# A decayed-attention stage taken two chunks at a time, followed by a three-pass matmul network

## The chip, the cores and the metric

The kernel runs on one core of a Trainium2 chip. The metric is the time of one execution on the device in microseconds (us): 280.35, the median of 3 runs (280.11 to 280.44). Engines are called as in the profile: PE is the matmul engine, PEld its weight loads, DVE the vector engine, ACT the scalar engine, POOL GpSimd, SP the engine that issues all the transfers here.

## What is computed

Attention over 2 batches, 8 heads, 768 positions and head size 64, without softmax. In the reference a block of 64 positions gives

```
intra = (q @ k.T * Dmask) @ v                  # Dmask[i, j] = lam ** (i - j), lower triangle
inter = (q * lam ** (pos + 1)) @ kv_state
out   = intra + inter
kv_state = lam ** block * kv_state + (k * lam ** (block - 1 - pos)).T @ v
```

and the state of a block goes into the next one. Two dense stages follow on x (1536 x 512). The first shifts by one token: `xk = mu_k*x + (1-mu_k)*x_prev`, `xr` likewise, `k = relu(xk @ w_k)` (512 to 1024), `v = k*k @ w_v`, `x = sigmoid(xr @ w_r) * v`. The second is `(sigmoid(conv5(x)) * (x @ w_val)) @ w_out`. Everything is float32.

## The kernel before

**Attention.** The kernel works in chunks of 128 positions: 6 chunks in each of 2 batches, n = 0 to 11. A chunk has four groups of matmuls on PE: `scores(n)` (S), `update(n)` (U, the product that goes into the state), `inter(n)` (I, query times state) and `attend(n)` (A, weighted scores times v). Chunks 0 and 6 begin a batch and have no I; chunks 5 and 11 end one and have no U. All operands have 64 rows or 64 columns somewhere, so the groups use PE cut into parts: S as 64*128, U and A as 128*64, I as 64*64 (the profile gives this shape in each row). Around them:

- POOL makes `kdec` (keys with decay, `decay_k`, needed by U) and `qd` (queries with decay, `decay_q`, needed by I).
- DVE multiplies the scores with the decay table (`weigh`, pT, two instructions, needed by A) and adds the next state (`new_state`, needed by the next I).
- ACT scales the old state first (`fade`, four instructions, needed by `new_state`) and copies the output of a chunk from PSUM to x (`evacuate_x`, needed before PE writes the same banks again).
- Each engine has one queue, in the order in which the code lists its work. PE's order is S(n+1), U(n), I(n), A(n). In the gaps ACT and DVE already mix the first 512 tokens (`mix_part`, `mix`, `mix_high`, `mix_low`) and split w_k into a high and a low part (`high`, `low`).
- S has two pairs of PSUM banks, U two banks, the output banks 4 and 5 (0 and 1 for the last chunk). kdec, qd, pT and state have two buffers each. Loaded chunks have 6 buffers (`IN_BUFS`), qk and kv of a chunk being one transfer of 512 KB each.

**Dense stages.** Each product is made of three matmuls of 128x512 (`three_pass`: high*high, high*low, low*high). For a block t of 512 tokens `hidden(t, n)` makes 8 groups of 12 matmuls, `receptance(t, m)` 4 groups, `value(t, m)` 4 groups of 24. `hidden(0, 0)` waits for all four pieces of the low part of w_k (`wk_lo` at 4). `receptance` waits for `xr_lo` and the squares that free its banks, `value` for 8 `kk_lo` and 4 `wv_lo`.

Of the kernel before, what the change touches and what calls it, by code (L numbers as in the profile page):

```python
# [29 lines left out]
IN_BUFS = 6  # L30
# [18 lines left out]
def build(nc, prm_in, qk_in, kv_in, w_k, w_v, w_r, w_val, w_out, out):  # L49
    with ExitStack() as ctx:  # L50
# [10 lines left out]
        def place(name, shape, at, dt=F32):  # L61
# [44 lines left out]
        in_at = [kk_at + i * 8 * KB for i in range(4)] + [ring_at, r_at]  # L106
        qk = [place(f"qk_{i}", [P, 2, DM], in_at[i]) for i in range(IN_BUFS)]
        kv = [place(f"kv_{i}", [P, 2, DM], in_at[i] + 4 * KB) for i in range(IN_BUFS)]
        pT = place("pT", [P, 2, 2, DM], xr_at)
        kdec = place("kdec", [P, 2, DM], xr_at + 8 * KB)  # L110
        qd = place("qd", [P, 2, DM], xr_at + 12 * KB)
        dec = place("dec", [P, H, CH], own_at)
        qdec = place("qdec", [P, PAIRS, CH], own_at + 4 * KB)
        state = place("state", [P, 2, PAIRS * D], own_at + 6 * KB)
        faded = place("faded", [P, PAIRS * D], own_at + 8 * KB)
        zeros = place("zeros", [P, CH], own_at + 9 * KB)
        warm = place("warm", [P, P], own_at + 10 * KB)
        spare = place("spare", [P, 1], own_at + 11 * KB)
        ident = place("ident", [P, P], own_at + 12 * KB)
# [5 lines left out]
        ps_s, ps_u = [[ps[:, 2 * i + j, :] for j in range(2)] for i in range(2)], [6, 7]  # L125
# [20 lines left out]
            sem(z) for z in "wk_hi wk_lo wr_hi wr_lo wv_hi wv_lo w2_hi w2_lo".split()]  # L146
        (xk_part, xk_full, xk_hi, xk_lo, xr_part, xr_full, xr_hi, xr_lo) = [
# [23 lines left out]
        def out_banks(n):  # L171

            return (0, 1) if n == NCH - 1 else (4, 5)
# [21 lines left out]
        def _(sp):  # L195
# [22 lines left out]
            load_qk(2)  # L218
            load_kv(1)
            load_qk(3)  # L220
            load_kv(2)
            load_kv(3)
            load_qk(4)
            load_kv(4)
            load_qk(5)
            load_kv(5)
            load_qk(6)
            load_kv(6)
            load_qk(7)
            load_weight(wk_raw, w_k, 0, wk_here)  # L230
            load_kv(7)
            load_qk(8)
            load_kv(8)
            load_weight(wk_raw, w_k, 1, wk_here)
            load_qk(9)
            load_kv(9)
            load_weight(wk_raw, w_k, 2, wk_here)
            load_qk(10)
            load_kv(10)
            load_qk(11)  # L240
            load_weight(wk_raw, w_k, 3, wk_here)
            load_kv(11)
            for i in range(2):
                load_weight(wr_raw, w_r, i, wr_here)
            for i in range(4):
                load_weight(wv_raw, w_v, i, wv_here)
# [19 lines left out]
        def _(pool):  # L266
            def decay_k(n):
                if has_update(n):
                    i = n % IN_BUFS
                    pool.wait_ge(kv_here[i], 16 * (n // IN_BUFS + 1))  # L270
                    if updates(n) > 2:
                        pool.wait_ge(update_done, updates(n) - 2)
                    nc.gpsimd.tensor_tensor(  # L273
                        kdec[:, updates(n) % 2, :].rearrange("p (h d) -> p h d", h=H),
                        kv[i][:, 0, :].rearrange("p (h d) -> p h d", h=H),
                        dec[:, :, CH - 1:CH].to_broadcast([P, H, D]), ALU.mult).then_inc(kdec_ready, 1)

            def decay_q(n):
                b, c = at(n)
                if c > 0:  # L280
                    i = n % IN_BUFS
                    pool.wait_ge(qk_here[i], 16 * (n // IN_BUFS + 1))  # L282
                    if inters(n) > 2:
                        pool.wait_ge(inter_done, inters(n) - 2)
                    nc.gpsimd.tensor_tensor(
                        qd[:, inters(n) % 2, :], qk[i][:, 0, :],
                        qdec[:, :, :].rearrange("p a i -> p (a i)"), ALU.mult).then_inc(qd_ready, 1)
# [11 lines left out]
            decay_k(0)  # L299
            pool.wait_ge(qdec_ok, PAIRS)  # L300
            decay_q(1)
            for n in range(1, NCH):
                decay_k(n)
                if n + 1 < NCH:
                    decay_q(n + 1)
# [4 lines left out]
        def _(act):  # L310
            def evacuate_x(n):
                b, c = at(n)
                cols = slice(b * SEG + HALO + c * CH, b * SEG + HALO + (c + 1) * CH)
                act.wait_ge(att_done, n + 1)
                first = out_banks(n)[0]
                nc.scalar.copy(x[:, :, cols].rearrange("p (g a) i -> p g a i", g=2),
                               ps[:, first:first + 2, 0:2 * CH].rearrange("p g (a i) -> p g a i", a=2)).then_inc(x_ready, 1)

            def fade(n):

                act.wait_ge(state_ready, updates(n - 1))
                for a in range(PAIRS):
                    cols = slice(a * D, (a + 1) * D)
                    nc.scalar.activation(faded[:, cols], state[:, n % 2, cols], ACT.Copy,
# [7 lines left out]
            def mix_part(t, k, which):  # L332

                to, done, free = ((xk_f, xk_part, h_done), (xr_f, xr_part, r_done))[which]
                act.wait_ge(x_ready, min(CT * (t + 1), NCH))
# [69 lines left out]
            evacuate_x(0)  # L405
            act.wait_ge(qdec_ok, PAIRS)
            fade(1)
            evacuate_x(1)
            fade(2)
            evacuate_x(2)  # L410
            fade(3)
            evacuate_x(3)
            fade(4)
            mix_part(0, 0, 0)
            mix_part(0, 1, 0)
            evacuate_x(4)
# [12 lines left out]
            evacuate_x(8)
            fade(9)  # L430
            high(wk, wk_raw, 1, wk_here, wk_hi)
            evacuate_x(9)
            fade(10)
            high(wk, wk_raw, 2, wk_here, wk_hi)
            evacuate_x(10)
            high(wk, wk_raw, 3, wk_here, wk_hi)
            evacuate_x(11)
# [58 lines left out]
        def _(dve):  # L496
            def weigh(n):

                dve.wait_ge(scores_done, n + 1)
                if n >= 2:  # L500
                    dve.wait_ge(att_done, n - 1)
                for row in range(2):
                    nc.vector.tensor_tensor(pT[:, n % 2, row, :], ps_s[n % 2][row],  # L503
# [3 lines left out]
            def new_state(n):  # L507
# [5 lines left out]
                if inters(n - 1) > 0:  # L513
                    dve.wait_ge(inter_done, inters(n - 1))
                to, got = state[:, (n + 1) % 2, :], ps[:, ps_u[updates(n) % 2], 0:PAIRS * D]
# [86 lines left out]
            for n in range(NCH):  # L602
                if n + 1 < NCH:
                    weigh(n + 1)
                new_state(n)
                if n == 4:
                    mix(0, 0, 0)
                    mix(0, 1, 0)
                if n == 5:
                    mix(0, 2, 0)  # L610
                    mix(0, 3, 0)
                if n == 6:
                    mix_low(0, 0, 0)
                if n == 7:
                    mix_low(0, 1, 0)
                    mix_low(0, 2, 0)
                if n == 8:
                    mix_low(0, 3, 0)
                    low(wk, wk_raw, 0, wk_hi, wk_lo)
                if n > 8:  # L620
                    low(wk, wk_raw, n - 8, wk_hi, wk_lo)
            for i in range(2):
                low(wr, wr_raw, i, wr_hi, wr_lo)
# [59 lines left out]
        def _(pe):  # L683
# [23 lines left out]
            def update(n):  # L707
# [7 lines left out]
                if u > 2:  # L715
                    pe.wait_ge(state_ready, u - 2)
                for a in range(PAIRS):
                    for row in range(2):
                        h, at_k = head_of(row, a), (row * PAIRS + a) * D
                        last = nc.tensor.matmul(ps[rows_of(row), ps_u[u % 2], a * D:(a + 1) * D],  # L720
                                                kdec[:, u % 2, at_k:at_k + D], kv[i][:, 1, h * D:(h + 1) * D],
# [3 lines left out]
            def place_of(n, row, a):  # L725
                return ps[rows_of(out_half(row, a)), out_banks(n)[a // 2], a % 2 * P:(a % 2 + 1) * P]

            def inter(n):
# [5 lines left out]
                if n < NCH - 1:  # L734
                    pe.wait_ge(x_ready, n)
                else:
                    pe.wait_ge(p_ready, 2 * n)
                for a in (0, 2, 1, 3):
                    for row in range(2):
                        last = nc.tensor.matmul(place_of(n, row, a), state[rows_of(row), n % 2, a * D:(a + 1) * D],  # L740
                                                qd[rows_of(row), inters(n) % 2, a * P:(a + 1) * P],
                                                start=(a % 2 == 0), stop=False, skip_group_check=True)
                last.then_inc(inter_done, 1)

            def attend(n):
# [4 lines left out]
                if c == 0 and n > 0:  # L750
                    pe.wait_ge(x_ready, n)
                for a in range(PAIRS):
                    for row in range(2):
                        h = head_of(row, a)
                        last = nc.tensor.matmul(place_of(n, row, a), kv[i][:, 1, h * D:(h + 1) * D],  # L755
                                                pT[:, n % 2, row, a * P:(a + 1) * P],
                                                start=(c == 0 and a % 2 == 0), stop=(a % 2 == 1), skip_group_check=True)
                last.then_inc(att_done, 1)

            def hidden(t, n):  # L760
                if n == 0:
                    pe.wait_ge(xk_lo, KT * (t + 1))
                    pe.wait_ge(wk_lo, 4)
                    if t == 0:
                        pe.wait_ge(p_ready, 2 * NCH)
                if t == 0 and n == 2:
                    pe.wait_ge(x_ready, NCH - 1)
                if t == 0 and n == 4:
                    pe.wait_ge(state_ready, updates(NCH - 1))
                if t == 0 and n == 6:  # L770
                    pe.wait_ge(x_ready, NCH)
# [4 lines left out]
                three_pass(ps[:, bank_of("mlp", t, n), :],  # L776
                           [(lambda z, k=k: wk[z][:, k * DF + n * P:k * DF + (n + 1) * P], lambda z, k=k: xk[z][:, k, :])
# [64 lines left out]
            scores(2)  # L842
            inter(1)
            attend(1)
            update(1)
            for n in range(2, NCH):
                if n + 1 < NCH:
                    scores(n + 1)
                update(n)
                inter(n)  # L850
                attend(n)
# [66 lines left out]
```

## Time and profile before

| | |
|---|---|
| Median of 3 runs | 280.35 us (280.11 to 280.44) |
| Profiled execution | 280.36 us, of which the span of the profile is 278.6 us |
| PE busy | 271.7 us (98%) |
| DVE, ACT, POOL busy | 166.7, 126.9, 35.1 us |
| Transfers | 22.83 MB, 17.46 MB of them in the first 75 us |
| First matmul of `hidden(0, 0)` | 47.12 us from the start of the span |

A span begins with the first instruction of the program that the profile shows. A row of a timeline gives the start, the duration, the engine, the line of the kernel, the operation, output<-input, the shape and count of the merged instructions, and in brackets the idle time of the engine before it with what ended it.

### The profile page before, as it was taken

Reading aid. Unit: us, or ns where it says so; the run is one execution under the profiler, and the core shown is the slowest. Engines: PE = TensorE matmul, PEld = TensorE weight load, DVE = VectorE, ACT = ScalarE, POOL = GpSimd, SP = SyncE. Lnnn points to the kernel's source line nnn. Section 1 sums busy time; section 2 is a strip of 40 time slices with the busy share of each in tenths; the row PEclk is TensorE's granted clock in tenths of the full one; section 3 lists DMA queues with packets and bytes.
Section 4 is the critical chain, followed back from the end, with each engine's and each line's share of the span. In section 5 each row is a group of like instructions: output and inputs, shape, how many; then the busy total and the mean of one; then the engine's idle time right before and its main releaser. Section 6 shows DMA issues by size and latency. Waiting matters only on the chain.

```text
span 278.6 us, 4270 instructions
## 1 busy us (share of the span) xinstructions
PE 271.7 (98%) x1740; PEld 226.0 (81%) x1740; DVE 166.7 (60%) x253; ACT 126.9 (46%) x229; POOL 35.1 (13%) x30
## 2 busy tenths in 40 slices
PE   8799998999999999999999999999999999999996
PEld 7688886888888888888888888888888888888885
DVE  5658998975976103456786635436987599415000
ACT  2337668867794114356821134558226404512121
POOL 1686660008600000000000000000000000000000
DMA  6999995000000000000000000260000000300223
GB/s 235 409 405 411 408 402 235 0 0 0 2 0 0 0 2 0 0 0 2 1 0 0 4 0 0 72 231 0 0 0 2 0 0 0 115 38 0 113 78 113
DMA packets 7506, 22.83 MB, mean 82 GB/s; under 512 B 960, under 2 KB 1216, under 8 KB 7488
## 3 DMA queue, kind: packets, MB, share of 16 engines
q1 hardware_dynamic: 7488, 22.57, 21.1%
q8 instruction: 14, 0.23, 0.3%
q14 instruction: 4, 0.03, 0.0%
HBM read 19.42 MB, written 3.15 MB: 81 GB/s over the span
## 4 chain that ended last, share of the span: by engine, by line
PE 95%; DMA 2%; issue 1%; SPq 0%; POOL 0%; ACT 0%; POOLq 0%
PE ps L687 27%; PE ps L688 27%; PE ps L689 27%; PE ps L703 4%; PE ps L755 4%; PE ps L740 2%; PE ps L720 2%; DMA kv<-in_kv 2%; POOL kdec L273 0%; SPq L204 0%; SPq L214 0%; ACT out_sb L400 0%; POOLq L282 0%; POOLq L270 0%
## 5 line engine op out<-in xcount | busy, mean ns | idle before, releaser
L687 PE MATMUL ps<-xk_h,wk_h 128*128 128x512 f32 x96 | 37.4, 390 | 0.8 <-issue 0.8
L689 PE MATMUL ps<-xk_h,wk_l 128*128 128x512 f32 x96 | 37.4, 389 | 0.0
L687 PE MATMUL ps<-kk_h,wv_h 128*128 128x512 f32 x96 | 37.3, 389 | 0.0
L688 PE MATMUL ps<-kk_l,wv_h 128*128 128x512 f32 x96 | 37.3, 389 | 0.0
L689 PE MATMUL ps<-kk_h,wv_l 128*128 128x512 f32 x96 | 37.3, 389 | 0.0
L688 PE MATMUL ps<-xk_l,wk_h 128*128 128x512 f32 x96 | 37.3, 389 | 0.0
L542 DVE SCALAR_TENSOR_TENSOR kk_f<-ps,ring 128x512 f32<-128x512 f32 x24 | 16.6, 691 | 29.0 <-ACT ring L353 29.0
L566 DVE SCALAR_TENSOR_TENSOR gate<-x,prm,gate 128x512 f32<-128x512 f32 x48 | 32.6, 747 | 0.0
L353 ACT ACTIVATE ring<-ps 128x512 f32<-128x512 f32 x24 | 14.3, 598 | 31.6 <-PE ps L689 31.5
L370 ACT ACTIVATE gate<-x,prm 128x512 f32<-128x512 f32 x12 | 8.7, 725 | 42.6 <-DVE x L552 42.6
L687 PEld LDWEIGHTS ps<-xk_h,wk_h 128*128 128x128 f32 x96 | 18.0, 188 | 4.7 <-issue 1.0
L687 PEld LDWEIGHTS ps<-kk_h,wv_h 128*128 128x128 f32 x96 | 18.0, 188 | 3.8
L688 PEld LDWEIGHTS ps<-kk_l,wv_h 128*128 128x128 f32 x96 | 18.0, 188 | 3.8
L688 PEld LDWEIGHTS ps<-xk_l,wk_h 128*128 128x128 f32 x96 | 18.0, 188 | 3.8
L689 PEld LDWEIGHTS ps<-xk_h,wk_l 128*128 128x128 f32 x96 | 18.0, 188 | 3.7
L689 PEld LDWEIGHTS ps<-kk_h,wv_l 128*128 128x128 f32 x96 | 18.0, 188 | 3.7
L552 DVE TENSOR_TENSOR x<-ps,r 128x512 f32<-128x512 f32 x12 | 8.3, 691 | 20.5 <-PE ps L689 20.5
L688 PE MATMUL ps<-w_l,gh 128*128 128x512 f32 (+1 forms) x52 | 19.4, 373 | 0.0
L689 PE MATMUL ps<-w_h,gl 128*128 128x512 f32 (+1 forms) x52 | 19.4, 373 | 0.0
L687 PE MATMUL ps<-w_h,gh 128*128 128x512 f32 (+1 forms) x52 | 19.4, 373 | 0.0
L503 DVE TENSOR_TENSOR pT<-ps,dec 128x512 f32<-128x512 f32 x24 | 15.4, 682 | 6.4 <-PE ps L703 6.3
L547 DVE TENSOR_TENSOR kk_l<-kk_f,kk_h 128x512 fp32r<-128x512 f32 x24 | 18.0, 752 | 1.8 <-ACT kk_h L357 1.8
(71 smaller groups left out, 507.5 us busy)
## 6 DMA issues: line engine op xcount, KB each, us to landing
qk<-in_qk SPq DMA_DIRECT2D x12, 512.0 KB, 10.2
kv<-in_kv SPq DMA_DIRECT2D x10, 512.0 KB, 11.0
out<-out_sb SPq DMA_DIRECT2D x11, 256.0 KB, 2.0
wk_raw<-in_w_k SPq DMA_DIRECT2D x4, 512.0 KB, 11.8
wv_raw<-in_w_v SPq DMA_DIRECT2D x4, 512.0 KB, 14.7
wr_raw<-in_w_r SPq DMA_DIRECT2D x2, 512.0 KB, 13.2
w_raw<-in_w_val SPq DMA_DIRECT2D x2, 512.0 KB, 4.4
w_raw<-in_w_out SPq DMA_DIRECT2D x2, 512.0 KB, 6.9
```

The costliest lines, as they stand in the source:

```text
L353: nc.scalar.activation(ring[:, n % 4, :], ps[:, bank_of("mlp", t, n), :], ACT.Relu).then_inc(relu_ready, 1)
L370: nc.scalar.activation(like(t, gate[t][:, k, :]), x_cols(t, k, HALO), ACT.Copy, scale=prm[:, col:col + 1]).then_inc(tap0, 1)
L503: nc.vector.tensor_tensor(pT[:, n % 2, row, :], ps_s[n % 2][row], dec[:, row * PAIRS:(row + 1) * PAIRS, :].rearrange("p a i -> p (a i)"), ...
L542: nc.vector.scalar_tensor_tensor(out=kk_f[:, n, :], in0=ps[:, bank_of("mlp", t, n), :], scalar=0.0, in1=ring[:, n % 4, :], op0=ALU.max, op ...
L547: nc.vector.tensor_tensor(kk[1][:, n, :], kk_f[:, n, :], f32(kk[0][:, n, :]), ALU.subtract).then_inc(kk_lo, 1)
L552: nc.vector.tensor_tensor(x_cols(t, m, 1), like(t, ps[:, bank_of("mlp", t, FT + KT + m), :]), like(t, r[:, m, :]), ALU.mult).then_inc(x2_r ...
L566: nc.vector.scalar_tensor_tensor(out=like(t, gate[t][:, k, :]), in0=x_cols(t, k, HALO - j), scalar=prm[:, col:col + 1], in1=like(t, gate[t ...
L687: nc.tensor.matmul(to, left(0), right(0), start=(i == 0), stop=False)
L688: nc.tensor.matmul(to, left(0), right(1), start=False, stop=False)
L689: done = nc.tensor.matmul(to, left(1), right(0), start=False, stop=(i == last))
L703: last = nc.tensor.matmul(ps_s[n % 2][row][:, cols], qk[i][rows_of(row), 1, cols], qk[i][rows_of(row), 0, cols], start=True, stop=True)
L755: last = nc.tensor.matmul(place_of(n, row, a), kv[i][:, 1, h * D:(h + 1) * D], pT[:, n % 2, row, a * P:(a + 1) * P], start=(c == 0 and a % ...
```

## The change

Attention goes by pairs of chunks. PE's order for pair p is S(2p+2), S(2p+3), I(2p), I(2p+1), U(2p+2), U(2p+3), A(2p), A(2p+1), so the updates of the next pair stand ahead of the output products of this one. kdec, qd, pT and state have four buffers, the chunks 8 (`IN_BUFS`), two of them and pT in the memory of w_v, whose load therefore waits for chunk 7. The two output banks hold a pair, and one copy takes it out. w_k is laid out so that its piece i has all rows of columns 256 i to 256 i + 255; piece 0 of its low part stays on DVE, pieces 1 to 3 and the low part of w_r go to POOL, and `hidden(0, n)` waits only for its own piece. The order of the queues changes with it:

```
 PE
             scores(0); scores(1); attend(0); update(0)
-            scores(2); inter(1); attend(1); update(1)
-            for n in range(2, NCH):
-                if n + 1 < NCH:
-                    scores(n + 1)
-                update(n); inter(n); attend(n)
+            update(1)
+            for p in range(NP):
+                if p + 1 < NP:
+                    scores(2 * p + 2); scores(2 * p + 3)
+                inter(2 * p); inter(2 * p + 1)
+                if p + 1 < NP:
+                    update(2 * p + 2); update(2 * p + 3)
+                if p > 0:
+                    attend(2 * p)
+                attend(2 * p + 1)
 update(n) waits
-                if u > 2:
-                    pe.wait_ge(state_ready, u - 2)
+                if n >= 2:
+                    pe.wait_ge(state_ready, updates(n - 2))
 inter(n) waits
-                if n < NCH - 1:
-                    pe.wait_ge(x_ready, n)
-                else:
-                    pe.wait_ge(p_ready, 2 * n)
+                if opens(n, True):
+                    pe.wait_ge(x_ready, n // 2)
 hidden(0, n) waits
-                    pe.wait_ge(wk_lo, 4)
+                if t == 0 and n == 0:
+                    pe.wait_ge(wk_lo_first, 1)
+                elif t == 0 and n % 2 == 0:
+                    pe.wait_ge(wk_lo, n // 2)
 DVE
+            weigh(1)
+            for p in range(NP):
+                new_state(2 * p)
+                if p + 1 < NP:
+                    weigh(2 * p + 2); weigh(2 * p + 3)
+                new_state(2 * p + 1)
+                if p == 2:
+                    mix(0, 0, 0); mix(0, 1, 0); mix(0, 2, 0)
+                if p == 3:
+                    mix(0, 3, 0); mix_low(0, 0, 0); mix_low(0, 1, 0)
+                if p == 4:
+                    mix_low(0, 2, 0); mix_low(0, 3, 0)
+                if p == 5:
+                    low(wk, wk_raw, 0, wk_hi, wk_lo_first)
-            for i in range(2):
-                low(wr, wr_raw, i, wr_hi, wr_lo)
 ACT
+            fade(1); evacuate_x(0); fade(2); fade(3); evacuate_x(1); fade(4)
+            for k in range(KT):
+                mix_part(0, k, 0)
+            evacuate_x(2); fade(7)
+            for k in range(3):
+                mix_high(0, k, 0)
+            fade(8); evacuate_x(3); fade(9); mix_high(0, 3, 0); fade(10); evacuate_x(4)
+            for i in range(3):
+                high(wk, wk_raw, i, wk_here, wk_hi)
+            evacuate_x(5); high(wk, wk_raw, 3, wk_here, wk_hi)
 POOL
+            decay_k(0); decay_k(1); decay_q(1)
+            for p in range(1, NP):
+                decay_k(2 * p); decay_k(2 * p + 1); decay_q(2 * p); decay_q(2 * p + 1)
+            for i in range(1, 4):
+                low(wk, wk_raw, i, wk_hi, wk_lo)
+            for i in range(2):
+                low(wr, wr_raw, i, wr_hi, wr_lo)
 SP
+            load_qk(0); load_qk(1); load_kv(0); load_kv(1)
+            for p in range(1, NP - 1):
+                load_qk(2 * p); load_qk(2 * p + 1); load_kv(2 * p); load_kv(2 * p + 1)
+            load_qk(NCH - 2); load_qk(NCH - 1)
+            load_weight(wk_raw, w_k, 0, wk_here)
+            load_kv(NCH - 2); load_kv(NCH - 1)
+            (then pieces 1 to 3 of w_k, w_r, and after att_done >= 8 the four of w_v)
```

The diff is cut here: several calls stand on one line, and the lines removed from the queues of DVE, ACT, POOL and SP are those of the kernel above. `evacuate_x(p)` copies banks 4 and 5 whole (1024 columns) after `att_done` 2p + 2.

## Rows read from the trace of the kernel before

**Rows 1.** The page: busy time, chain that ended last, its shares by engine.
```profile
PE 271.7 (98%) x1740; PEld 226.0 (81%) x1740; DVE 166.7 (60%) x253; ACT 126.9 (46%) x229; POOL 35.1 (13%) x30
PE 95%; DMA 2%; issue 1%; SPq 0%; POOL 0%; ACT 0%; POOLq 0%
```

**Rows 2.** Stretches: length; busy us of PE, PEld, DVE, ACT, POOL; clock, DMA share, GB/s.
```profile
14.90:46.30 31.40, 30.77 (x560) 25.45 (x560) 26.97 (x38) 20.00 (x47) 18.38 (x15) 1.00 1.00 396
47.10:80.00 32.90, 32.88 (x145) 27.24 (x146) 25.24 (x32) 24.77 (x40) 10.22 (x4) 1.00 0.01 1
```

**Rows 3.** PE's timeline, the groups on which the prices rest.
```profile
8.55 1.09 PE L755 MATMUL ps<-pT,kv 128*64 128x128 f32 x16 [1.44 <-DMA kv<-in_kv]
...
17.12 1.77 PE L703 MATMUL ps<-qk 64*128 64x128 f32 x16
...
28.49 0.69 PE L720 MATMUL ps<-kv,kdec 128*64 128x64 f32 x16
29.00 1.05 PE L755 MATMUL ps<-pT,kv 128*64 128x128 f32 x16
29.98 1.16 PE L703 MATMUL ps<-qk 64*128 64x128 f32 x16
...
33.69 1.16 PE L703 MATMUL ps<-qk 64*128 64x128 f32 x16
34.78 0.69 PE L720 MATMUL ps<-kv,kdec 128*64 128x64 f32 x16
35.40 0.67 PE L740 MATMUL ps<-qd,state 64*64 64x128 f32 x16
35.99 1.09 PE L755 MATMUL ps<-pT,kv 128*64 128x128 f32 x16
37.02 1.16 PE L703 MATMUL ps<-qk 64*128 64x128 f32 x16
...
45.10 1.23 PE L755 MATMUL ps<-pT,kv 128*64 128x128 f32 x16
47.12 0.47 PE L687 MATMUL ps<-xk_h,wk_h 128*128 128x512 f32 x1 [0.78 <-issue]
...
79.88 0.39 PE L687 MATMUL ps<-kk_h,wv_h 128*128 128x512 f32 x1
```

**Rows 4.** POOL's timeline: waits for transfers, and its long instruction.
```profile
13.73 1.06 POOL L273 TENSOR_TENSOR kdec<-kv,dec 128x512 f32<-128x512 f32 x1 [0.28 <-DMA kv<-in_kv]
...
26.24 1.06 POOL L273 TENSOR_TENSOR kdec<-kv,dec 128x512 f32<-128x512 f32 x1 [1.28 <-DMA kv<-in_kv]
27.53 1.64 POOL L285 TENSOR_TENSOR qd<-qk,qdec 128x512 f32<-128x512 f32 x1 [0.23 <-DMA qk<-in_qk]
...
63.17 2.42 POOL L292 TENSOR_TENSOR wv_l<-wv_raw,wv_h 128x1024 fp32r<-128x1024 f32 x1 [21.82 <-ACT wv_h L330]
```

**Rows 5.** DVE's timeline: weigh, state, and a mix beside POOL and alone.
```profile
27.95 1.77 DVE L527 SCALAR_TENSOR_TENSOR xk_f<-x,om,xk_f 128x512 f32<-128x512 f32 x1
...
42.80 1.28 DVE L503 TENSOR_TENSOR pT<-ps,dec 128x512 f32<-128x512 f32 x2
44.00 0.41 DVE L520 TENSOR_TENSOR state<-faded,ps 128x256 f32<-128x256 f32 x1
...
45.79 1.22 DVE L538 TENSOR_TENSOR wk_l<-wk_raw,wk_h 128x1024 fp32r<-128x1024 f32 x1 [0.25 <-ACT wk_h L330]
...
50.22 2.73 DVE L527 SCALAR_TENSOR_TENSOR xr_f<-x,om,xr_f 128x512 f32<-128x512 f32 x4
...
74.50 0.68 DVE L547 TENSOR_TENSOR kk_l<-kk_f,kk_h 128x512 fp32r<-128x512 f32 x1
```

**Rows 6.** ACT's timeline: copy out of PSUM, fade, cast of twice the width.
```profile
33.81 0.59 ACT L316 COPY x<-ps 128x512 f32<-128x512 f32 x1 [0.95 <-PE ps L755]
34.30 1.06 ACT L324 ACTIVATE faded<-state,qdec 128x64 f32<-128x64 f32 x4
35.26 1.03 ACT L330 CAST wk_h<-wk_raw 128x1024 fp32r<-128x1024 f32 x1
```

More of the change, by code:

```diff
@@ L103, in build @@
         out_sb = [place(f"out_sb_{t}", [P, CT, DM], gate_at[t]) for t in range(NT)]
-        in_at = [kk_at + i * 8 * KB for i in range(4)] + [ring_at, r_at]
+        in_at = [kk_at + i * 8 * KB for i in range(4)] + [ring_at, r_at, wv_at + 16 * KB, wv_at + 24 * KB]
         qk = [place(f"qk_{i}", [P, 2, DM], in_at[i]) for i in range(IN_BUFS)]
         kv = [place(f"kv_{i}", [P, 2, DM], in_at[i] + 4 * KB) for i in range(IN_BUFS)]
-        pT = place("pT", [P, 2, 2, DM], xr_at)
-        kdec = place("kdec", [P, 2, DM], xr_at + 8 * KB)
-        qd = place("qd", [P, 2, DM], xr_at + 12 * KB)
+        pT = place("pT", [P, 4, 2, DM], wv_at)
+        kdec = place("kdec", [P, 4, DM], xr_at)
+        qd = place("qd", [P, 4, DM], xr_at + 8 * KB)
         dec = place("dec", [P, H, CH], own_at)
         qdec = place("qdec", [P, PAIRS, CH], own_at + 4 * KB)
[L114 to L119, printed above, removed]
+        state = place("state", [P, 4, PAIRS * D], own_at + 6 * KB)
+        faded = place("faded", [P, PAIRS * D], own_at + 10 * KB)
+        zeros = place("zeros", [P, CH], own_at + 11 * KB)
+        warm = place("warm", [P, P], own_at + 11 * KB + 512)
+        spare = place("spare", [P, 1], own_at + 12 * KB)
+        ident = place("ident", [P, P], own_at + 12 * KB + 512)
         prm = place("prm", [P, PRM], prm_at)
@@ L124, in build @@
         ps = ctx.enter_context(nc.psum_tensor("ps", [P, 8, 512], F32))
-        ps_s, ps_u = [[ps[:, 2 * i + j, :] for j in range(2)] for i in range(2)], [6, 7]
+        ps_s, ps_o, ps_u = [[ps[:, 2 * i + j, :] for j in range(2)] for i in range(2)], [4, 5], [6, 7]
         f32 = lambda z: z.bitcast(F32)
@@ L169, in inters, with has_inter, opens @@
             return n - n // NCB
-        def out_banks(n):
-            return (0, 1) if n == NCH - 1 else (4, 5)
+        def has_inter(n):
+            return at(n)[1] > 0
+        def opens(n, of_state):
+            if not has_inter(n):
+                return n == 0 and not of_state
+            return of_state and (n % 2 == 0 or not has_inter(n - 1)) and n != 1
         def x_cols(t, k, back, of=x):
@@ L299, in _ @@
             decay_k(0)
+            decay_k(1)
             pool.wait_ge(qdec_ok, PAIRS)
             decay_q(1)
-            for n in range(1, NCH):
-                decay_k(n)
-                if n + 1 < NCH:
-                    decay_q(n + 1)
+            for p in range(1, NP):
+                decay_k(2 * p)
+                decay_k(2 * p + 1)
+                decay_q(2 * p)
+                decay_q(2 * p + 1)
+            for i in range(1, 4):
+                low(wk, wk_raw, i, wk_hi, wk_lo)
+            for i in range(2):
+                low(wr, wr_raw, i, wr_hi, wr_lo)
             for i in range(4):
@@ L323, in fade @@
                     cols = slice(a * D, (a + 1) * D)
-                    nc.scalar.activation(faded[:, cols], state[:, n % 2, cols], ACT.Copy,
+                    nc.scalar.activation(faded[:, cols], state[:, n % 4, cols], ACT.Copy,
                                          scale=qdec[:, a, CH - 1:CH]).then_inc(faded_ready, 1)
@@ L719, in update @@
                         h, at_k = head_of(row, a), (row * PAIRS + a) * D
-                        last = nc.tensor.matmul(ps[rows_of(row), ps_u[u % 2], a * D:(a + 1) * D],
-                                                kdec[:, u % 2, at_k:at_k + D], kv[i][:, 1, h * D:(h + 1) * D],
+                        last = nc.tensor.matmul(ps[rows_of(row), ps_u[n % 2], a * D:(a + 1) * D],
+                                                kdec[:, n % 4, at_k:at_k + D], kv[i][:, 1, h * D:(h + 1) * D],
                                                 start=True, stop=True, skip_group_check=True)
@@ L725, in place_of @@
             def place_of(n, row, a):
-                return ps[rows_of(out_half(row, a)), out_banks(n)[a // 2], a % 2 * P:(a % 2 + 1) * P]
+                first = a % 2 * 2 * P + n % 2 * P
+                return ps[rows_of(out_half(row, a)), ps_o[a // 2], first:first + P]
             def inter(n):
@@ L733, in inter @@
                 pe.wait_ge(state_ready, updates(n - 1))
-                if n < NCH - 1:
-                    pe.wait_ge(x_ready, n)
-                else:
-                    pe.wait_ge(p_ready, 2 * n)
+                if opens(n, True):
+                    pe.wait_ge(x_ready, n // 2)
                 for a in (0, 2, 1, 3):
                     for row in range(2):
-                        last = nc.tensor.matmul(place_of(n, row, a), state[rows_of(row), n % 2, a * D:(a + 1) * D],
-                                                qd[rows_of(row), inters(n) % 2, a * P:(a + 1) * P],
-                                                start=(a % 2 == 0), stop=False, skip_group_check=True)
+                        last = nc.tensor.matmul(place_of(n, row, a), state[rows_of(row), n % 4, a * D:(a + 1) * D],
+                                                qd[rows_of(row), n % 4, a * P:(a + 1) * P],
+                                                start=(opens(n, True) and a % 2 == 0), stop=False, skip_group_check=True)
                 last.then_inc(inter_done, 1)
@@ L755, in attend, with wk_col @@
                         last = nc.tensor.matmul(place_of(n, row, a), kv[i][:, 1, h * D:(h + 1) * D],
[L756 to L757 removed]
+                                                pT[:, n % 4, row, a * P:(a + 1) * P],
+                                                start=(opens(n, False) and a % 2 == 0),
+                                                stop=(a % 2 == 1 and n % 2 == 1), skip_group_check=True)
                 last.then_inc(att_done, 1)
+            def wk_col(k, n):
+                return n // 2 * PIECE + k * 2 * P + n % 2 * P
             def hidden(t, n):
@@ L901 @@
         "kv": np.stack([tokens(k[:, order]), tokens(v)], axis=2),
-        "w_k": by_rows(np.asarray(inputs["moe_w_k"])),
+        "w_k": by_columns(np.asarray(inputs["moe_w_k"])),
         "w_v": by_rows(np.asarray(inputs["moe_w_v"])),
```

147 lines of the change are left out of this document (54 added, 93 removed).

## The prediction

> **What bounds the kernel now.** I read the page first: PE is busy 98% of the span and holds 95% of the chain that ended last [rows 1]. That says little about the attention stage, because a busy PE is not PE at its peak. Then the stretches: from 47.1 us on, PE is full without a break at a granted clock of 1.00 [rows 2], so what follows `hidden(0, 0)` is a block of fixed length. The change can move the end only by moving the start of `hidden(0, 0)`, 47.12 us [rows 3], or by starving a later group. Third, PE's timeline up to there, which gives the price of a group, and last the timelines of POOL, DVE and ACT, to see what each group of the new order would wait for.
>
> In PE's timeline the distance from one group's start to the next is what counts. Chunk 8 shows it whole: S 33.69, U 34.78, I 35.40, A 35.99, next S 37.02 [rows 3]. That is 1.09 + 0.62 + 0.59 + 1.03 = 3.33 us, with PE never idle. Chunk 6 has no I, so A follows U in the same shape (128*64): U then takes 0.51 (28.49 to 29.00) and A 0.98 (29.00 to 29.98) [rows 3]. So the change of shape between two groups costs 0.11 + 0.05 = about 0.15 us. It is PE work in no group, and a "busy" row hides it. Without it I take S 0.90, U 0.46, I 0.45, A 0.88, together 2.69; four changes make 0.64, the one into S being the dearest (I take 0.20). A further cost is a pause of about 0.3 us once in some 7.6 groups, such as S at 17.12 with 1.77 instead of 1.16 [rows 3]; I spread it as 0.04 to 0.05 per group.
>
> `hidden(0, 0)` starts 0.78 after PE ran dry [rows 3]. The profile names no releaser, but the last `wk_l` on DVE ends at 45.79 + 1.22 = 47.01, 0.11 before it [rows 5]: that wait is the low part of w_k.
>
> **The change, step by step.**
>
> *Changes of shape (gain).* Counted in the code up to the first `hidden`: 40 before; 19 after (three in each of pairs 0 to 4, two in pair 5, one before A(0), one before `hidden`). 21 fewer times 0.15 is -3.2 us. Bounds: only the changes between U, I and A are seen without their switch. If those into and out of S cost nothing, 11 of the saved ones remain, -1.65; at 0.20 each it is -4.2. I take 0.15, since the sum 3.33 closes with it.
>
> *The wait for w_k's low part (gain).* Up to -0.8: only piece 0 is needed for `hidden(0, 0)`. It goes in full only if piece 0 is ready, which comes out below.
>
> *Start of the new order (loss).* U(1) now stands ahead of S(2), and U(2), U(3) ahead of A(1), so PE waits for keys and their decay. kdec of chunk 2 began at 13.73, when its kv had landed, and that of chunk 7 at 26.24, 10 transfers later in the queue's order: 1.25 us per transfer [rows 4]. In the new order kv of chunk 1 takes the place of qk 2, three places ahead of kv of chunk 2: 13.7 - 3 x 1.25 = 9.9. kdec takes 1.06 [rows 4] and PE starts 0.14 after it. U(1) thus at 11.05 (PE is free at 10.3: wait 0.75), S(2), S(3) 11.7 to 13.7, I(1) to 14.3. kv of chunk 2 keeps its place, 13.7: U(2) at 13.7 + 1.06 + 0.14 = 14.9 (wait 0.45); chunk 3 lands at 15.0, U(3) at 16.2 (wait 0.75), A(1) to 17.7. S(4) starts at 17.8 against 17.12 [rows 3]: 0.7 behind. New waits: 1.95. They can't be below 1.2 (kv of chunk 3 alone) if the transfers keep their pace.
>
> *Pairs 1 and 2 (work, no real wait).* A full pair is 2 x 2.69 + 0.50 for three changes + 0.3 for the pause = 6.2 us, against 6.95 for two chunks before. Pair 1 lacks U(5): 17.8 to 23.5. Pair 2: to 29.7. The new copy of a whole pair has no row: 512 columns take 0.59, a cast of 1024 against 512 adds 0.43 (1.03, and 0.60 for 512), so 1.02 [rows 6]; ends of the range 0.59 and 1.2 (two copies). It starts 0.25 after A, and the next I needs it 2.0 later, behind two S: hidden. But ACT queues `fade(2)` behind `evacuate_x(0)`: 17.95 to 18.95, fade 1.06 [rows 6] to 19.9, state 0.41 [rows 5] to 20.35, I(3) at 20.45. PE would want it at 20.4: cover just used up. The same for `evacuate_x(1)`, `fade(4)`, state 4 at 26.1, I(5) at 26.2. Without that cover each microsecond on ACT is one on PE.
>
> *Pair 3 (loss, the largest).* DVE must give, in its order, weigh(6), weigh(7), three mixes, the state of chunk 6, weigh(8), weigh(9), the state of chunk 7. The state of chunk 4 ends at 26.1; two weighs of 1.20 each [rows 5] end at 28.4. A mix alone takes about 0.68 (2.73 for four), but 1.77 when it starts beside POOL's 27.53 instruction [rows 4, 5]. POOL makes kdec of chunks 8 and 9 just then: their kv are two and three transfers behind chunk 7's in the count (28.7, 30.0). So the three mixes end at 31.75, not at 30.4. State 6 is there at 32.15; I(7), wanted at 31.8, waits 0.4. The two weighs run 32.1 to 34.5, state 7 to 34.9. U(9) waits for state 7 because its bank is that of U(7): PE wants it at 33.45 and gets 35.0, wait 1.55. Behind U(9) stand A(6) and A(7), whose inputs have long been ready, and SP's transfers of w_v, which nobody misses. Bounds of the two waits together: 0.9 (mixes never blocked) and 2.6 (each mix blocked by 1.0 more). Pair 3 ends at 37.4 and pair 4, lacking U(11), at 43.05.
>
> *Pair 5 (loss).* No S is left to cover the copy. I(10) needs banks 4 and 5: A(9) ends at 43.05, the copy goes 43.3 to 44.3, I(10) starts at 44.4, wait 1.3. ACT has `fade(10)` ahead of it until 42.7, so that is not in the way. Bounds 0.9 (a copy of 0.59) and 1.6. I(10), I(11), A(10), A(11) end at 47.4. `wk_hi` of piece 0 follows the copy, 45.25, and DVE's low part is there at 46.5, before PE: the old wait is gone in full.
>
> *Behind 47 us.* The layout of w_k changes addresses alone: nothing, with hidden's matmuls as cover. Pieces 1 to 3 and both of w_r on POOL take 2.42 each [rows 4]: first at 46.2, w_k done by 53.5, needed from 53.0 (piece 1, done 48.7) on, so in time; w_r done near 59, needed at 69. Removed from DVE: five of 1.22. w_v's four transfers start after A(7), 37.4, and need 5; POOL first used one at 63.17 [rows 4]. Cost taken: nothing; the third rival says what if not.
>
> *The sum.* -3.2 (changes) - 0.8 (w_k) + 1.95 (start) + 0.4 + 1.55 (pair 3) + 1.3 (pair 5) = +1.2. The old order had waits of its own in this stretch that go (U(2) for its kdec, I(11) for state), together about 0.3, and one pause of 0.3 falls into a new wait. Left: +0.6, so `hidden(0, 0)` at 47.7. The profiled execution, 280.36, stands 0.01 from the median, and the change gives 280.36 + 0.6 = 281.0 us.
>
> **A rule of the Trainium skill.** The row first: a mix took 1.77 beside POOL's instruction of 27.53, and 0.68 apiece alone [rows 4, 5]. The Trainium skill (SBUF — State Buffer, section Who interferes with whom) says that a VectorE instruction with two SBUF inputs is fully blocked by a GpSimd instruction that reads SBUF, and the other way round; by that rule the trace agrees. Were there no such block, the same walk would put `hidden(0, 0)` at 46.7.
>
> **The rivals.**
>
> *DVE keeps ahead (faster).* Place: the three mixes of pair 3. For it: they are short alone, and POOL's instructions start with the landing of kv, whose time I know to some 0.3. Against: one of the four mixes before collided in the same way [rows 5]. It decides if the mixes end by about 30.4: then I(7) does not wait, U(9) waits 0.9, and `hidden(0, 0)` comes at 46.6: 279.8 us, 0.2% faster than before.
>
> *The savings and the waits cancel.* If a change of shape costs 0.18 on the mean instead of 0.15 (S is unseen without one), the gain grows by 0.6: 280.4 us, the same.
>
> *DVE falls behind POOL after 47 us (slower still).* Place: `value(0, 0)`, at 79.88 before, with the last `kk_l` at 75.2 [rows 3, 5]: a margin of 4.7. POOL gets five more instructions of 2.42, and each mix, `xr_l` and `kk_l` may wait for one. The xr mixes begin at 52.2 and end at 60 instead of 53; alternating with w_v's pieces the last `kk_l` ends near 79.1, against PE at 80.4. The margin is 1.3 us. One more block of 2.4 gives a wait of 1.1, and so 282.1 us. By the rule of the page named above this block is full-length each time, which is what the walk assumed.
>
> *The pairs break the chain of ACT (slower).* If the copy takes 1.2 and not 1.02, I(3), I(5), I(10) come later by 0.2 each and U(9) with them: 281.8.
>
> **How the numbers follow.** About 0.2% (0.56 us) is what a measurement of this kernel can tell from no change. The forecast, 281.0, lies just past it. Chances: forecast 0.40; DVE ahead 0.17; cancel 0.18; POOL behind 47 us 0.13; ACT's chain 0.12. The forecast and its near surroundings reach from 280.5 to 281.5, so part of it counts as the same: I give 0.15 of its 0.40 there. That makes slower 0.25 + 0.13 + 0.12 = 0.50, the same 0.15 + 0.18 = 0.33, faster 0.17. The range takes in the first rival with a mix in hand and the third: 279.6 to 282.4. Changes of shape at 0.20 throughout (-1.0) and the upper bounds of pair 3 (+0.6) lie within it.
>
> **What would show it right or wrong.** Right: S(4) near 17.8; U(1), U(2), U(3) behind kdec; U(9) behind state 7 with 1.5 us; I(10) behind the copy with 1.3; `hidden(0, 0)` near 47.7 with no wait for `wk_l`; A after U at 0.88 per group without a change. Wrong: mixes of 0.7 each at 28 to 31 us; S after S above 1.0; a wait ahead of `value(0, 0)` or `receptance(0, 0)`; or transfers off the pace of 1.25, which would move the first 18 us.

## The result, and the profile after

| | before | after |
|---|---|---|
| Median | 279.84 us (16 runs, 279.37 to 281.12) | 281.14 us (16 runs, 280.25 to 282.41) |
| Profiled execution | 280.36 us, span 278.6 | 281.85 us, span 279.7 |
| First matmul of `hidden(0, 0)` | 47.12 | 48.23 |
| First matmul of `value(0, 0)` | 79.88 | 81.01 |

The changed kernel is 0.48% slower: ratio 1.0048, 95% interval 1.0036 to 1.0059, some 1.3 us. The forecast was 281.0, range 279.6 to 282.4. The kernel before was timed again beside it, and its median is 0.5 us under the 280.35 of the first three runs. So the forecast of the time came within 0.14 us, but in part by luck: it was a change of +0.6 us on a base that was 0.5 too high, and the change measured is +1.3, twice as much.

PE's timeline of the changed kernel answers to [rows 3] (L694 is S, L730 I, L711 U, L743 A, L678 the first matmul of hidden):

```profile
9.69 0.69 PE L711 MATMUL ps<-kv,kdec 128*64 128x64 f32 x16 [0.21 <-POOL kdec L270]
10.90 0.69 PE L711 MATMUL ps<-kv,kdec 128*64 128x64 f32 x16 [0.53 <-POOL kdec L270]
...
14.70 0.69 PE L711 MATMUL ps<-kv,kdec 128*64 128x64 f32 x16 [0.53 <-issue]
15.97 0.69 PE L711 MATMUL ps<-kv,kdec 128*64 128x64 f32 x16 [0.59 <-POOL kdec L270]
...
17.46 2.06 PE L694 MATMUL ps<-qk 64*128 64x128 f32 x32
19.45 1.45 PE L730 MATMUL ps<-qd,state 64*64 64x128 f32 x32
20.83 0.69 PE L711 MATMUL ps<-kv,kdec 128*64 128x64 f32 x16
21.34 1.92 PE L743 MATMUL ps<-pT,kv 128*64 128x128 f32 x32
23.19 2.06 PE L694 MATMUL ps<-qk 64*128 64x128 f32 x32
...
32.27 0.81 PE L730 MATMUL ps<-qd,state 64*64 64x128 f32 x16 [0.80 <-issue]
33.01 0.69 PE L711 MATMUL ps<-kv,kdec 128*64 128x64 f32 x16
35.03 0.69 PE L711 MATMUL ps<-kv,kdec 128*64 128x64 f32 x16 [1.34 <-DVE state L513]
...
39.38 0.66 PE L730 MATMUL ps<-qd,state 64*64 64x128 f32 x14
40.91 0.81 PE L730 MATMUL ps<-qd,state 64*64 64x128 f32 x18 [0.87 <-issue]
...
45.30 1.10 PE L730 MATMUL ps<-qd,state 64*64 64x128 f32 x32 [1.21 <-ACT x L319]
46.33 1.97 PE L743 MATMUL ps<-pT,kv 128*64 128x128 f32 x32
48.23 0.50 PE L678 MATMUL ps<-xk_h,wk_h 128*128 128x512 f32 x1
```

Two A of a pair take 1.85 from start to start (21.34 to 23.19), where two alone took 2 x 1.03 before: the changes of shape are saved. What is new stands in the brackets: U(1), U(2) and U(3) wait for kdec, I(7) for state 6, U(9) for state 7, I(10) for the copy. Three brackets name no releaser ("issue"). For two of them another row gives it: POOL's kdec of chunk 2 ran from 13.54 to 14.60, just ahead of U(2) at 14.70, and DVE's state 6 ended at 31.75 + 0.41 = 32.16, just ahead of I(7) at 32.27. The third has none in any queue: 0.87 us inside I(8), after its 14th matmul. DVE and ACT show what I(7), U(9) and I(10) waited for:

```profile
28.15 3.68 DVE L520 SCALAR_TENSOR_TENSOR xk_f<-x,om,xk_f 128x512 f32<-128x512 f32 x3
31.75 0.41 DVE L510 COPY state<-ps 128x256 f32<-128x256 f32 x1
32.09 2.47 DVE L496 TENSOR_TENSOR pT<-ps,dec 128x512 f32<-128x512 f32 x4
34.48 0.40 DVE L513 TENSOR_TENSOR state<-faded,ps 128x256 f32<-128x256 f32 x1
...
52.86 8.31 DVE L520 SCALAR_TENSOR_TENSOR xr_f<-x,om,xr_f 128x512 f32<-128x512 f32 x4 [5.51 <-ACT xr_f L344]
...
80.17 0.68 DVE L540 TENSOR_TENSOR kk_l<-kk_f,kk_h 128x512 fp32r<-128x512 f32 x1
```

```profile
44.14 1.01 ACT L319 COPY x<-ps 128x1024 f32<-128x1024 f32 x1 [1.29 <-PE ps L743]
```

The three mixes take 3.68 us (2.0 alone), because POOL's kdec of chunks 8 and 9 run beside them at 28.77 and 30.03. Behind the hidden start nothing changed: from there to `value(0, 0)` it is 32.78 us after and 32.76 before. So the later `hidden(0, 0)`, 1.11 us, is all of the difference of the spans (279.71 - 278.55 = 1.16).

### The profile page after: what moved, and what is told of

The parts are those of the page before. It is cut to its first block, busy times and chain, and to the rows that moved or that the text cites. A ratio compares the mean times of both kernels' runs of the same rounds, so it can differ in the third digit from the quotient of the medians.

```text
span 279.7 us, 4257 instructions
## 1 busy us (share of the span) xinstructions
PE 268.5 (96%) x1740; PEld 224.8 (80%) x1740; DVE 169.2 (60%) x248; ACT 125.6 (45%) x223; POOL 49.7 (18%) x35
## 2 busy tenths in 40 slices
DMA packets 7506, 22.83 MB, mean 82 GB/s; under 512 B 960, under 2 KB 1216, under 8 KB 7488
## 4 chain that ended last, share of the span: by engine, by line
PE 88%; DMA 3%; DVE 3%; issue 2%; ACT 1%; SPq 1%; POOL 1%; DVEq 0%; POOLq 0%
PE ps L678 27%; PE ps L680 27%; PE ps L679 27%; DMA kv<-in_kv 3%; PE ps L743 3%; DVE pT L496 1%; PE ps L694 1%; PE ps L730 1%; PE ps L711 1%; DVE xk_f L520 1%; POOL kdec L270 1%; ACT x L319 1%; SPq L211 1%; ACT faded L327 0%; SPq L216 0%
## 5 line engine op out<-in xcount | busy, mean ns | idle before, releaser
L678 PE MATMUL ps<-xk_h,wk_h 128*128 128x512 f32 x96 | 37.5, 390 | 0.0
L680 PE MATMUL ps<-kk_h,wv_l 128*128 128x512 f32 x96 | 37.4, 389 | 0.0
L680 PE MATMUL ps<-xk_h,wk_l 128*128 128x512 f32 x96 | 37.4, 389 | 0.0
L679 PE MATMUL ps<-xk_l,wk_h 128*128 128x512 f32 x96 | 37.4, 389 | 0.0
L679 PE MATMUL ps<-kk_l,wv_h 128*128 128x512 f32 x96 | 37.4, 389 | 0.0
L678 PE MATMUL ps<-kk_h,wv_h 128*128 128x512 f32 x96 | 37.3, 389 | 0.0
L540 DVE TENSOR_TENSOR kk_l<-kk_f,kk_h 128x512 fp32r<-128x512 f32 x24 | 21.2, 883 | 1.8 <-ACT kk_h L360 1.8
L678 PEld LDWEIGHTS ps<-xk_h,wk_h 128*128 128x128 f32 x96 | 18.0, 188 | 3.8 <-issue 0.2
L678 PEld LDWEIGHTS ps<-kk_h,wv_h 128*128 128x128 f32 x96 | 18.0, 188 | 3.8 <-DVE kk_l L540 0.2
L678 PE MATMUL ps<-w_h,gh 128*128 128x512 f32 (+1 forms) x52 | 19.4, 373 | 0.0
L680 PE MATMUL ps<-xr_h,wr_l 128*128 128x512 f32 x48 | 18.7, 389 | 0.0
L678 PE MATMUL ps<-xr_h,wr_h 128*128 128x512 f32 x48 | 18.7, 389 | 0.0
```

The costliest lines, as they stand in the source:

```text
L540: nc.vector.tensor_tensor(kk[1][:, n, :], kk_f[:, n, :], f32(kk[0][:, n, :]), ALU.subtract).then_inc(kk_lo, 1)
L678: nc.tensor.matmul(to, left(0), right(0), start=(i == 0), stop=False)
L679: nc.tensor.matmul(to, left(0), right(1), start=False, stop=False)
L680: done = nc.tensor.matmul(to, left(1), right(0), start=False, stop=(i == last))
```

## The experiments

Theory 1: the end is set by what PE waits for ahead of `hidden(0, 0)`, and each of these waits can be taken away by itself. Theory 2: the margin at `value(0, 0)` (81.01, the last `kk_l` ends 80.85) is spent, so an earlier hidden start would be lost there. Theory 3 came up with the first four runs and concerns the pause without a releaser: it sits at a fixed number of PE's instructions and waits for a packet of them. Times are compared by medians. A profile is one execution, and executions differ in their start: A(0), which waits for a transfer, began between 7.46 and 9.02 us.

**Outputs ahead of updates.**

```
-                if p + 1 < NP:
-                    update(2 * p + 2)
-                    update(2 * p + 3)
                 if p > 0:
                     attend(2 * p)
                 attend(2 * p + 1)
+                if p + 1 < NP:
+                    update(2 * p + 2)
+                    update(2 * p + 3)
```

> The changed kernel with A(2p), A(2p+1) ahead of U(2p+2), U(2p+3) in each pair. The number of changes of shape stays the same. Theory 1 (the order of the updates makes PE wait: U(2) and U(3) for kdec, U(9) for the state of chunk 7; the outputs, whose inputs are ready, can fill those waits, and their copy starts earlier): hidden(0,0) at 45.0 instead of 48.2, no wait of U(9), I(10) waits 0.8 instead of 1.2, time 3.2 us below the changed kernel, 278.0. Rival (the updates stand first because the states are late otherwise: I(2p+1) then waits for fade and state): waits of 0.5 or more at I(3), I(5), I(9), a gain below 1 us.

278.27 us, ratio to the kernel before 0.9947 (0.9929 to 0.9965): 2.9 us under the changed kernel and 1.5 under the one before. Its PE timeline around U(8) to U(10) and I(10):

```profile
34.22 1.10 PE L711 MATMUL ps<-kv,kdec 128*64 128x64 f32 x32
35.25 2.06 PE L694 MATMUL ps<-qk 64*128 64x128 f32 x32
37.24 0.66 PE L730 MATMUL ps<-qd,state 64*64 64x128 f32 x14
38.34 0.81 PE L730 MATMUL ps<-qd,state 64*64 64x128 f32 x18 [0.45 <-issue]
39.09 1.97 PE L743 MATMUL ps<-pT,kv 128*64 128x128 f32 x32
40.88 0.64 PE L711 MATMUL ps<-kv,kdec 128*64 128x64 f32 x16
42.26 1.10 PE L730 MATMUL ps<-qd,state 64*64 64x128 f32 x32 [0.74 <-ACT x L319]
...
45.64 0.50 PE L678 MATMUL ps<-xk_h,wk_h 128*128 128x512 f32 x1
```

U(8) and U(9) run as one block without a wait, I(10) waits 0.74 (expected 0.8), and no I waits for a state. The rival falls. The order of the updates, and not the pairing, made the kernel slow. The hidden start came at 45.64, not 45.0. The rows hold waits that the expectation had not: pauses of 0.58 in I(4) and 0.45 here, and 0.81 of S(5) for its queries at 17.95.

**The last pair in banks of its own.** The edit is condensed here; `hidden(0, 2)` then waits for the copy of pair 4 and `hidden(0, 6)` for that of pair 5.

```
+   (ps_o if n < NCH - 2 else [0, 1])[a // 2]        # place_of; the copy likewise
-   if opens(n, True):            pe.wait_ge(x_ready, n // 2)
+   if opens(n, True) and n < NCH - 2: pe.wait_ge(x_ready, n // 2)
+   elif n >= NCH - 2:            pe.wait_ge(p_ready, 2 * (NCH - 1))
```

> The changed kernel with the outputs of the last pair in banks 0 and 1, so that I(10) no longer waits for the copy of pair 4. Theory 1 (the start of hidden(0,0) sets the end): I(10) starts at 44.1 instead of 45.3, hidden(0,0) at 47.4 (then piece 0 of the low part of w_k, ready at 47.35, sets it), time 0.8 us below the changed kernel, 280.3. Theory 2 (the margin at value(0,0) is used up: its last kk_l ended 80.85 and it began at 81.01, and that chain hangs on ACT and POOL, which do not get earlier by more than the 0.36 that ACT waited for A(11)): hidden(0,0) earlier by 0.8 all the same, but value(0,0) waits 0.4 to 0.5, and the time falls by 0.3 to 0.4 only.

**The same, with the low parts of w_k and w_r on DVE.** The two loops of `low` go from POOL's list to DVE's, behind piece 0.

> As the run before (outputs of the last pair in banks 0 and 1), with pieces 1 to 3 of the low part of w_k and both of w_r back on DVE. Theory 1: same as the run before, 280.3, as POOL's work does not matter. Theory 2 (POOL's long instructions block DVE's mixes and kk_l before value(0,0)): the xr mixes take 2.7 instead of 8.3 us, the last kk_l ends near 76, value(0,0) does not wait, the whole 0.8 us arrives: 280.3 here and 280.7 in the run before.

280.87 (ratio 1.0032, 1.0017 to 1.0047) and 281.19 (1.0037, 1.0022 to 1.0053), against 1.0048 of the changed kernel: the intervals overlap, so the 0.8 us that both theories had promised of one run or the other did not come in either. PE's timeline of the second:

```profile
42.75 1.10 PE L733 MATMUL ps<-qd,state 64*64 64x128 f32 x32
43.78 1.75 PE L746 MATMUL ps<-pT,kv 128*64 128x128 f32 x26
46.52 0.60 PE L746 MATMUL ps<-pT,kv 128*64 128x128 f32 x6 [0.99 <-issue]
47.05 0.50 PE L679 MATMUL ps<-xk_h,wk_h 128*128 128x512 f32 x1
```

I(10) no longer waits, but PE stands still 0.99 us inside A(11), where the changed kernel had no pause. From S(10) to `hidden(0, 0)` it is 10.71 and 11.20 us in these two runs and 10.84 in the changed kernel: the pause took back nearly all of the wait in the first and more than it in the second. Theory 2 falls in these executions: in the first run `value(0, 0)` came 32.79 us after `hidden(0, 0)`, no later than ever, and with the low parts on DVE the last `kk_l` ended at 75.11 instead of 80.85 and the time did not fall. What POOL's long instructions did is there in the first run all the same (the four xr mixes 8.43 us, 2.73 in the second); it cost nothing here.

**The layout of w_k alone, in the kernel before.** `by_columns` for w_k, `pe.wait_ge(wk_lo, n // 2 + 1)` for each even n; all else as before.

> The kernel before with one part of the change alone: w_k laid out by columns and hidden(0,n) waiting for its own piece of the low part; the chunks go one by one, all low parts stay on DVE. Theory 1 (the 0.78 us of idle PE ahead of hidden(0,0) was the wait for the last piece of the low part): hidden(0,0) at 46.4 instead of 47.1, time 0.75 us below the kernel before. Rival (the wait was for something else, the mixed tokens or the last weigh, or the pause of PE's sequencer): no difference.

279.28 us, ratio 0.9977 (0.9965 to 0.9989): 0.6 us faster, near the 0.75 expected of a wait of 0.78. In its profile `hidden(0, 0)` follows A(11) at 46.80 with no idle time between them.

**State 7 ahead of weigh(9).** `new_state(2p+1)` between the two weighs.

> The changed kernel with new_state(2p+1) between weigh(2p+2) and weigh(2p+3) on DVE. Theory (U(9) waits because state 7 stands behind two weighs of 1.2 us on DVE): the wait of U(9), 1.34 us after, falls to 0.3 or less, hidden(0,0) comes 1.0 to 1.2 us earlier and the time with it, 280.0. Rival (state 7 is bound by fade(7) on ACT, which starts when state 6 is there, 31.75 + 0.41, and takes 1.06): then it can start at 33.3 at the earliest, which is just before PE wants it at 33.5, so the two agree on this run unless the copy of pair 2 delays the fade; a gain below 0.5 would say so.

280.14 us, ratio 1.0005 (0.9994 to 1.0016), 1.0 us under the changed kernel; U(8) and U(9) are one block of x32 at 33.23. This shows the U(9) wait as the forecast had it: its cause is the place of state 7 on DVE's queue, and it is worth 1.0 us of time.

**All three.** Outputs first, own banks, low parts on DVE.

> Outputs ahead of updates in each pair, the last pair in banks 0 and 1, the low parts of w_k and w_r on DVE. Theory 1 (waits add up): the run with the outputs first had 0.75 us of idle PE at I(10); it goes, hidden(0,0) at 45.0, 277.7. Theory 3 (PE's pauses sit at fixed numbers of instructions, 256 apart, and wait for a 16 KB packet of instructions that ends 1.3 us before PE resumes; PE that gets there earlier only waits longer): the pause at the 714th matmul, inside A(11), opens to 0.5 or more, and the gain over the run with the outputs first is below 0.3: 278.0 to 278.3.

278.35 us, ratio 0.9937 (0.9923 to 0.9952), the same as outputs first alone (278.27). Theory 1 alone is too simple, theory 3 came close with 278.0 to 278.3: the wait at I(10) went and a pause of 0.81 opened in A(11). Its PE timeline at the last two pauses:

```profile
36.39 0.66 PE L733 MATMUL ps<-qd,state 64*64 64x128 f32 x14
37.77 0.38 PE L733 MATMUL ps<-qd,state 64*64 64x128 f32 x2 [0.72 <-issue]
...
42.12 1.75 PE L746 MATMUL ps<-pT,kv 128*64 128x128 f32 x26
44.67 0.60 PE L746 MATMUL ps<-pT,kv 128*64 128x128 f32 x6 [0.81 <-issue]
45.20 0.50 PE L679 MATMUL ps<-xk_h,wk_h 128*128 128x512 f32 x1
```

**Six more changes of shape.** In that kernel S(2p+2), I(2p), S(2p+3), I(2p+1).

> As the run before, with PE's order S(2p+2), I(2p), S(2p+3), I(2p+1) in each pair: the same matmuls, six more changes of shape (two each in pairs 1, 2 and 4). Theory 1 (a change of shape costs 0.15 to 0.2 us of PE wherever it stands): hidden(0,0) and the time 0.8 to 1.1 us later than in the run before. Theory 3: some of it falls into the pauses, 0.3 to 0.8 us later. Rival (the changes cost nothing by themselves, the gaps between groups being semaphores and weight loads that come anyway): no difference.

279.12 us, ratio 0.9974 (0.9961 to 0.9987), 0.77 us above the run without: 0.13 us for a change, close to the 0.15 that the rows of before had given. The rival (no cost) falls; between theories 1 and 3 the number does not decide. In the profiles `hidden(0, 0)` is only 0.24 later, since pauses differ. Pair 2 has no pause in either: from S(6) to A(4) it took 3.38 us against 3.02, so 0.18 for each of its two changes.

**Added waits, to move the pauses.** In the version with all three edits, 32 and then 64 of them; then 32 in the kernel before.

```
             for _ in range(WARM): nc.tensor.matmul(...)
+            for _ in range(PADS): pe.wait_ge(warm_ok, 1)     # PADS = 32
```

> As the run with all three edits, with 32 more wait instructions on a semaphore long reached, on PE between its warm-up and S(0), where PE waits for a transfer anyway. Theory 3 (a pause stands at every 256th instruction of PE): the pauses at the matmuls number 342, 466, 590 and 714 move 16 matmuls forward, to 326, 450, 574 and 698. Rival (a pause belongs to a place in the work, such as the group before it or the transfers of that time): they stay. The time may go either way by up to 0.5 us.

> All three edits with 64 instead of 32 added waits on PE. In the run with 32 they made 16 instructions, and the last two pauses moved from the matmuls number 590 and 714 to 582 and 706. Theory 3: 64 waits make 32 instructions and put them at 574 and 698. Rival: they stay at 582 and 706, or at 590 and 714. The time may go either way by 0.5 us against 277.7.

> The kernel before with the 32 added waits alone. Theory 3: its pause at matmul 590 (0.16 us of idle) moves to 582; the order of chunks one by one hides most of each pause, so the time stays within 0.5 us of the kernel before. Rival (the gain of 0.7 us that the waits brought to the version with all edits has to do with the start of PE and not with the pauses): the same gain of 0.7 us here, 279.2.

The same pause in I(8) with 32 added waits, and just ahead of I(8) with 64:

```profile
35.28 0.44 PE L734 MATMUL ps<-qd,state 64*64 64x128 f32 x6
36.62 0.59 PE L734 MATMUL ps<-qd,state 64*64 64x128 f32 x13 [0.90 <-issue]
```

```profile
36.27 1.50 PE L696 MATMUL ps<-qk 64*128 64x128 f32 x23
38.60 0.37 PE L696 MATMUL ps<-qk 64*128 64x128 f32 x1 [0.82 <-issue]
38.90 0.56 PE L734 MATMUL ps<-qd,state 64*64 64x128 f32 x12
```

The 32 waits became 16 instructions (79 wait instructions of PE in the trace, 63 without them), so the pauses moved by 8 matmuls and not by the 16 I had written: from the matmuls number 590 and 714 (counted from 0) to 582 and 706. With 64 they stand at 575 and 699, as expected but for one; in the kernel before with 32 waits again at 582 and 706. Counted in instructions of PE (a weight load and a matmul each, and its waits) they stand at 1216 and 1472 within one, whatever the work there. The rival, that a pause belongs to a place in the work, falls.

The times: 277.67 with 32 (ratio 0.9940, 0.9909 to 0.9971; seven runs 277.2 to 278.4, two at 280.6 and 280.8), 278.07 with 64 (0.9952), and 280.73 for the kernel before with 32 (1.0027, 1.0007 to 1.0046), slower, not 0.7 faster. Theory 3 had expected that last one within 0.5 us of the kernel before; it is 0.8 off by the medians, 0.2 to 1.3 by the interval. Its profiled execution has I(7) waiting 1.16 for state 6, behind mixes that took 3.02 and 3.05 us for two instead of 2.36 and 2.43; why the median rose stays open. With 64 waits four of the eleven runs lie at 279.7 to 280.7, the profiled one among them. So the added waits don't help by themselves, and whether 32 of them help the combined version is not settled: the intervals overlap.

**The low parts on DVE, nothing else.**

> The changed kernel with pieces 1 to 3 of the low part of w_k and both of w_r back on DVE, and nothing else. Theory 1: the end is set before hidden(0,0), whose start doesn't move; the last kk_l ends 5 us earlier and nobody waits for it: the time stays, 281.1. Rival (the margin of 0.17 us at value(0,0) is lost in part of the executions, and POOL costs time there): up to 0.5 us less.

280.67 us, ratio 1.0033 (1.0022 to 1.0044) against 1.0048 (1.0036 to 1.0059). The median is 0.5 lower, the intervals overlap. Its profile has the same pause in I(8) and the same wait at I(10); `hidden(0, 0)` is 0.32 earlier all the same, as U(9) waited 0.79 and not 1.34. Whether some executions of the changed kernel lose a little at `value(0, 0)`, with a margin of 0.16, stays open; it is at most 0.5 us.

## Why the prediction was right

*The changes of shape* (-3.2): right in mechanism and size, 0.15 taken, 0.13 measured over six by the times and 0.18 by the rows, and 1.85 for two A. Pair 2 of the changed kernel took 6.23 us (23.19 to 29.42), forecast 6.2.

*The wait for w_k's low part* (-0.8): right. Alone it gave 0.6 us.

*The start* (+1.95): U(1), U(2), U(3) expected at 11.05, 14.9, 16.2 and there at 10.90, 14.70, 15.97, S(4) at 17.46 instead of 17.8. The three waits came to 1.65. The transfers kept their pace, and kdec of chunks 1 to 3 began 0.15 to 0.2 sooner than reckoned.

*Pair 3* (+0.4 and +1.55): I(7) waited 0.80 and U(9) 1.34, together 2.14 for 1.95; U(9) expected at 35.0, there at 35.03. The mixes, blocked by POOL as assumed, ended at 31.83, expected 31.75. Moving state 7 up in the queue gave 1.0 us. That the time of U(9) came out to 0.03 is luck: in three other profiles with this same order (own banks, with and without the low parts on DVE, and the low parts alone) the mixes took 2.87 to 2.88 us and U(9) waited 0.36, 0.24 and 0.79.

*Pair 5* (+1.3): the copy of 1024 columns took 1.01 to 1.02, the estimate 1.02; wait 1.21. But taking this wait away gave little or nothing, since a pause took its place. The price was right as a wait and wrong as a gain to be had.

*The pauses* (0.3 each, spread, one of them hidden): the mis-sized term. By the distances between starts, I(8) and I(9) took 41.65 - 39.38 = 2.27 us where I(10) and I(11), without a pause, took 46.33 - 45.30 = 1.03. The pause thus cost 1.24 (0.87 of it shown as idle), 0.94 more than the 0.3 forecast. Pair 3 ended at 37.39 (forecast 37.4), pair 4 at 44.09 instead of 43.05, and the last pair took 2.93 instead of 3.0, so this one pause is all of the lateness. The prediction's own row should have warned: S at 17.12 with 1.77 instead of 1.16 is a pause of 0.6, not 0.3. In the old order the pause at the same instruction cost 39.16 - 38.11 - 0.62 = 0.43. And the walk through the pairs ended at 47.4 while the sum gave 47.7; measured from the walk the start at 48.23 is 0.83 late, from the sum 0.53.

*Behind 47 us* (0): right in the end, with less to spare than worked out. The last `kk_l` ended at 80.85 instead of 79.1, the margin was 0.16 and not 1.3; the xr mixes took 8.31 us.

*Rivals.* "DVE keeps ahead" did not happen in the changed kernel's profile but was the right lever: the run with state 7 moved brought the kernel back to the one before. Its condition alone is not enough, though: in the run with own banks and low parts on DVE the mixes ended at 30.29 and U(9) waited 0.24, and `hidden(0, 0)` still came at 47.05 and not 46.6, with longer pauses. "The savings and the waits cancel" fell with the time, +1.3 us. "DVE falls behind POOL" came within 0.16 us of happening.

The loss of the changed kernel is thus its order, above all: with the outputs ahead of the updates the same pairs are 0.53% faster than the kernel before instead of 0.48% slower. A block of long-ready work (A, A) stood behind a wait (U(9), U(2), U(3)).

## What to carry to other kernels

When groups are regrouped to save switching, put the group whose inputs are long ready in front of the one that waits for another engine: here that order alone was worth 2.9 us, and the regrouping paid only with it. Read the queue of each helper engine in the new order and ask what stands ahead of the one instruction that PE waits for. A wait that is removed is a gain only if no other limit lies just behind it: a pause without a releaser in the trace deserves its own experiment before its time is spread as a tax.

## What the runs showed of the hardware

PE pauses at fixed numbers of its instructions, 256 apart (705, 961, 1216, 1472 in the traces), idle for 0.1 to 1.2 us, in the stage where its instructions are short. At the same spacing in the dense stages (a matmul starts every 0.227 us) no pause shows. Each pause has one packet of 16384 bytes on the queue that the profile names "instruction", 64 bytes for each of 256 instructions as worked out. The packet ends 1.2 to 1.6 us ahead of PE's resuming: it ended at 37.50 and PE resumed at 38.95 before, 39.60 and 40.91 after, 45.20 and 46.52 in the run with own banks and low parts on DVE, 36.98 and 38.34 with the outputs first. The DMA view of the changed kernel from 38.4 to 39.7 us shows the packet among the transfers:

```profile
q1 hardware_dynamic: 136, 0.50, 96.1%
q8 instruction: 1, 0.02, 5.3%
```

From the packet's start (36.39 before, 38.49 after) to PE's resuming at this instruction it is 2.3 to 2.6 us in all 13 traces, whether PE stood long or hardly at all. The pause is what PE does not fill of that stretch. From matmul to matmul at number 590 (582 and 575 with the added waits) it is 0.10 to 0.50 in the three traces of the old order, and 0.72 to 1.41 in the ten with pairs: 0.38 before, 1.14 after, 1.41 in the run with own banks and low parts on DVE. So a PE that arrives sooner only stands longer, as far as the packet does not start sooner with it.

The saturated transfers do not make the packet itself long: it took 1.11 us beside them, and 0.88 us at 71.46 and 1.29 us at 99.88, where it is the only packet in its window. What starts the packet was not tried, and neither was a way to start it sooner.
